# Up projections of two MLPs on one core: seven block products in Strassen's manner in place of eight

## What is computed

```python
qn = q / (norm(q, axis=1) + 1e-06); kn = k / (norm(k, axis=1) + 1e-06)
a = softmax(kn.transpose(0, 2, 1) @ qn / tau)      # 256 x 256 for each batch
x = (v @ a).reshape(12160, 256)
for w_in, w_out in ((moe_w_in, moe_w_out), (moe2_w_in, moe2_w_out)):
    x = np.maximum(x @ w_in, 0.0) ** 2 @ w_out
```

## Time and profile before

| | us |
|---|---|
| median of 3 runs | 2197.58 |
| lowest, highest | 2196.02, 2198.31 |
| the profiled execution | 2196.81 |
| its span, first to last instruction | 2194.7 |
| PE, DVE, ACT busy in the span | 2179.6, 1252.9, 1018.1 |

### The profile page before, as it was taken

One profiled execution on the slowest core, in us unless ns is written; L12 is line 12 of the kernel. 1 busy time (PEld: TensorE's weight loads), 2 busy tenths in 40 slices (PEclk: granted clock), 3 DMA queues, 4 the chain that ended last, 5 costly groups with the idle time before them and its releaser, 6 DMA issues.

```text
span 2194.7 us, 29614 instructions
## 1 busy us (share of the span) xinstructions
PE 2179.6 (99%) x9836; PEld 1826.6 (83%) x9836; DVE 1252.9 (57%) x1875; ACT 1018.1 (46%) x1722; POOL 3.2 (0%) x10
## 2 busy tenths in 40 slices
PE   8999999999999999999999999999999999999998
PEld 7888888888888888888888888888888888888887
DVE  6765555555565555656655555555555555555544
ACT  5554444444444454444544444444444444444443
POOL 0000000000000000000000000000000000000000
PEclk9999999999999999999999999999999999999999
DMA  8310001100011000112111010110110101101001
GB/s 294 96 49 20 19 19 25 33 19 19 19 29 29 19 19 20 33 23 49 37 20 19 1 20 0 19 19 0 19 18 1 19 0 19 19 0 18 10 1 19
DMA packets 215874, 60.94 MB, mean 28 GB/s; under 512 B 199281, under 2 KB 203377, under 8 KB 215825
## 3 DMA queue, kind: packets, MB, share of 16 engines
q1 hardware_dynamic: 215824, 60.31, 11.7%
HBM read 47.84 MB, written 12.45 MB: 27 GB/s over the span
## 4 chain that ended last, share of the span: by engine, by line
PE 99%; DVE 0%; DMA 0%; ACT 0%; issue 0%; DVEq 0%; SPq 0%
PE bank L321 32%; PE bank L323 32%; PE bank L322 32%; PE bank L455 2%; PE bank L402 0%; DMA qk<-in_k 0%; PE bank L416 0%; DVE s_acc L818 0%; PE bank L410 0%; DVE stats L822 0%; DVE rawl L713 0%; DVE out_sb L726 0%; ACT s_acc L592 0%; ACT rawh L521 0%; DVEq L90 0%
## 5 line engine op out<-in xcount | busy, mean ns | idle before, releaser
L747 DVE TENSOR_TENSOR g_sb<-r_sb 128x512 f32<-128x512 f32 (+1 forms) x768 | 527.3, 687 | 896.6 <-ACT r_sb L545 890.4
L545 ACT ACTIVATE r_sb<-bank 128x512 f32<-128x512 f32 (+1 forms) x768 | 456.0, 594 | 1109.3 <-PE bank L323 1102.1
L713 DVE TENSOR_TENSOR gl<-g_sb,gh 128x512 fp32r<-128x512 f32 (+1 forms) x768 | 519.7, 680 | 0.5 <-DVE g_sb L747 0.5
L533 ACT ACTIVATE gh<-r_sb 128x512 fp32r<-128x512 f32 (+1 forms) x768 | 470.7, 619 | 0.0
L321 PE MATMUL bank<-yh,w2h 128*128 128x512 f32 (+1 forms) x768 | 297.8, 388 | 0.0
L321 PE MATMUL bank<-xh,w1h 128*128 128x512 f32 (+1 forms) x768 | 297.4, 387 | 0.0
L322 PE MATMUL bank<-yl,w2h 128*128 128x512 f32 (+1 forms) x768 | 297.4, 387 | 0.0
L322 PE MATMUL bank<-xl,w1h 128*128 128x512 f32 (+1 forms) x768 | 297.4, 387 | 0.0
L321 PE MATMUL bank<-gh,o2h 128*128 128x512 f32 (+1 forms) x768 | 297.3, 387 | 0.0
L323 PE MATMUL bank<-yh,w2l 128*128 128x512 f32 (+1 forms) x768 | 297.3, 387 | 0.0
L323 PE MATMUL bank<-gh,o2l 128*128 128x512 f32 (+1 forms) x768 | 297.3, 387 | 0.0
(11 more groups left out here) (101 smaller groups left out, 1623.8 us busy)
## 6 DMA issues: line engine op xcount, KB each, us to landing
v_sb<-in_v SPq DMA_DIRECT2D x88, 128.0 KB, 3.0
out<-out_sb SPq DMA_DIRECT2D x88, 128.0 KB, 2.5
raw<-in_q SPq DMA_DIRECT2D x22, 256.0 KB, 2.7
raw<-in_k SPq DMA_DIRECT2D x22, 256.0 KB, 3.0
qk<-in_q SPq DMA_DIRECT2D x10, 512.0 KB, 5.2
qk<-in_k SPq DMA_DIRECT2D x10, 512.0 KB, 6.3
w_early<-in_moe_w_in SPq DMA_DIRECT2D x4, 512.0 KB, 6.0
xT<-in_moe_w_out SPq DMA_DIRECT2D x4, 512.0 KB, 3.9
```

Source lines behind the costliest of these rows:

```text
L533: nc.scalar.activation(gh[:, f % SLOTS, 0:n], r_sb[:, f % 2, 0:n], ACT.Square).then_inc(gh_done, 1)
L545: nc.scalar.activation(r_sb[:, f % 2, 0:n], h_ps[f % SLOTS][:, 0:n], ACT.Relu)\
L713: return nc.vector.tensor_tensor(dst, x, as32(hi), ALU.subtract)
L747: nc.vector.tensor_tensor(g_sb[:, f % 2, 0:n], r, r, ALU.mult).then_inc(sq_done, 1)
```

## The change

The kernel is written anew around a product of 2 x 2 blocks. A **unit** is two tiles of tokens (six units to a batch and layer: five of 2 x 512 and one of 2 x 480 tokens), 24 in all. The first layer of both batches comes first, its output goes to HBM (`y_mid`) and comes back for the second layer. SBUF holds the weights of one layer and batch at a time. A unit goes through eight **periods**; a period is one **chunk** of weights: block c of the first 1024 hidden features and block c of the second 1024. Its up product is a 2 x 2 block matrix of weights (128 x 128 blocks) times a 2 x 2 block matrix of activations, done with seven block products in place of eight (the Winograd form of Strassen's): four sums of weight blocks and four of activation blocks are made first, and each product is three matmuls as before. P1, P6, P7 and P4 add up in one bank, `ps_a`, and ACT copies its value out between them, since the partial sums are wanted too; P2 goes to `ps_b`, P5 and P3 to `ps_c`. The blocks are then C11 = P2 + copy 1 and C12 = P3 + copy 2 and C22 = P5 + copy 3 (adds on DVE), and C21 is the bank after P4. Each C is squared with relu, split, and goes down with 6 matmuls into two of four banks `y_ps`.

The four products of `ps_a` stand apart in the period, with down products of the period before and other up products between. Down work of period k-1 runs in period k. Other work is placed in slots of fixed periods (k counts periods, p is its place in the unit, u the unit):

- **weights**: the chunks for the first unit of a layer or batch are prepared one in a period, in periods 0 to 6, 47 to 54 and 95 to 102 (`w_chunk`): fold (4 float32 matmuls, batches only), `combine_w` (4 sums of 128 columns), `split_w` (896 columns, ACT then DVE). The next period's `p1` waits for it. The down weights are split in periods 0 to 7 and 96 to 103, and `d11` waits for them.
- **tokens**: the next unit's v is transposed at p = 2 and 3 and its sums are made at p = 3 and 4, its seven blocks split at p = 4 to 6. A half of v comes in 8 DMAs of 64 KB in place of 4 of 128.
- **batch 1's logits**: at p = 0, 1, 2, 4, 6, 7 of units 1 to 4, as 4 plain float32 matmuls on the unsplit data, added up in PSUM (bank 7) and not in SBUF; the squares are added at p = 2, 4 and 6 as DVE's last item. There is one buffer for q and k, as before.
- no loops: all 192 periods are straight-line code.

The core of the diff (on SyncE, the loads, stores and their places are left out; they are told above):

```diff
-            def up(kind, c, f, n):
-                wait(pe, relu_done, c - SLOTS + 1)
...
-                for cb in range(CB):
-                    cols = slice(f * P, (f + 1) * P)
-                    mm = three(h_ps[f % SLOTS][:, 0:n], wh_[:, cb, cols], wl_[:, cb, cols],
-                               ah[:, cb, 0:n], al[:, cb, 0:n], cb == 0, cb == CB - 1)
-                mm.then_inc(up_done, 1)
+            def product(m, ps, Q, first):
...
+                nc.tensor.matmul(ps[:, 0:n], wsh[:, c, cols], ah, start=first, stop=False, skip_group_check=not first)
+                nc.tensor.matmul(ps[:, 0:n], wsh[:, c, cols], al, start=False, stop=False, skip_group_check=not first)
+                return nc.tensor.matmul(ps[:, 0:n], wsl[:, c, cols], ah, start=False, stop=True,
+                                        skip_group_check=not first)
+            def p1(Q):
+                wait(pe, c21_relu, Q)
...
+                if c == 0:
+                    pe.wait_ge(x_lo, len(PIECES) * (u + 1))
+                if u % PAIRS == 0 and u <= LAYER:
+                    pe.wait_ge(w_lo, (u // PAIRS) * QUADS + c + 1)
+                product(0, ps_a, Q, True).then_inc(p1_done, 1)
+            def p2(Q):
+                wait(pe, c11_added, Q)
+                product(1, ps_b, Q, True).then_inc(p2_done, 1)
+            def p6(Q):
+                pe.wait_ge(p1_copied, Q + 1)
+                product(5, ps_a, Q, False).then_inc(p6_done, 1)
+            def p5(Q):
+                wait(pe, c12_added, Q)
+                product(4, ps_c, Q, True).then_inc(p5_done, 1)
+            def p7(Q):
+                pe.wait_ge(u_copied, Q + 1)
+                product(6, ps_a, Q, False).then_inc(p7_done, 1)
+            def p4(Q):
+                pe.wait_ge(v_copied, Q + 1)
+                product(3, ps_a, Q, False).then_inc(p4_done, 1)
+            def p3(Q):
+                pe.wait_ge(c22_added, Q + 1)
+                product(2, ps_c, Q, False).then_inc(p3_done, 1)
...
+            for k in range(PERIODS + 1):
+                up, dn = k < PERIODS, k > 0
+                if up:
+                    p1(k)
+                if dn:
+                    d11(k - 1)
+                beside(k)
+                if up:
+                    p2(k)
+                    p6(k)
+                if dn:
+                    d22(k - 1)
+                if up:
+                    p5(k)
+                    p7(k)
+                if dn:
+                    d21(k - 1)
+                if up:
+                    p4(k)
+                if dn:
+                    d12(k - 1, 0)
+                    d12(k - 1, 1)
+                if up:
+                    p3(k)
```

ScalarE and VectorE after, each period:

```diff
+                if dn:
+                    square21(k - 1)
+                if up:
+                    copy_p1(k)
+                if dn:
+                    high(k - 1, G21, F21, c21_sq, d21_done, g21_hi)
+                if p == 1 and u > 0:
+                    take_y(u - 1, 1)
+                if dn:
+                    high(k - 1, G12, F12, c12_sq, d12_done, g12_hi)
+                beside_early(k)
+                if up:
+                    copy_u(k)
+                    high(k, G11, F11, c11_sq, d11_done, g11_hi)
+                beside_mid(k)
+                if up:
+                    copy_v(k)
+                if p == 0 and u > 0:
+                    take_y(u - 1, 0)
+                beside_late(k)
+                if up:
+                    relu21(k)
+                    high(k, G22, F22, c22_sq, d22_done, g22_hi)
...
+                if dn:
+                    add12(k - 1)
+                    square(k - 1, F12, c12_added, c12_sq)
+                    g_low(k - 1, G22, F22, g22_hi, g22_lo)
+                if up:
+                    add11(k)
+                    square(k, F11, c11_added, c11_sq)
+                if dn:
+                    g_low(k - 1, G21, F21, g21_hi, g21_lo)
+                    g_low(k - 1, G12, F12, g12_hi, g12_lo)
+                beside_early(k)
+                if up:
+                    g_low(k, G11, F11, g11_hi, g11_lo)
+                beside_mid(k)
+                if up:
+                    add22(k)
+                    square(k, F22, c22_added, c22_sq)
+                beside_late(k)
```

More of the change, by code:

```diff
@@ new lines, in down @@
+            def down(Q, g, half, t, d, first, last):
+                u, c = divmod(Q, QUADS)
+                n = width(u)
+                ps, cols = y_ps[d, t][:, 0:n], slice(d * P, (d + 1) * P)
+                nc.tensor.matmul(ps, oh[:, half, c, cols], gh[:, g, 0:n], start=first, stop=False)
+                nc.tensor.matmul(ps, oh[:, half, c, cols], gl[:, g, 0:n], start=False, stop=False)
+                return nc.tensor.matmul(ps, ol[:, half, c, cols], gh[:, g, 0:n], start=False, stop=last)
@@ new lines, in d22, with d21 @@
+            def d22(Q):
+                u, c = divmod(Q, QUADS)
+                pe.wait_ge(g22_lo, Q + 1)
+                if c == 0:
+                    wait(pe, y1_taken, u)
+                down(Q, G22, 1, 1, 0, c == 0, False)
+                down(Q, G22, 1, 1, 1, c == 0, False).then_inc(d22_done, 1)
+            def d21(Q):
+                c = Q % QUADS
+                pe.wait_ge(g21_lo, Q + 1)
+                down(Q, G21, 1, 0, 0, False, c == QUADS - 1)
+                down(Q, G21, 1, 0, 1, False, c == QUADS - 1).then_inc(d21_done, 1)
@@ new lines, in d12, with raw_logits @@
+            def d12(Q, d):
+                c = Q % QUADS
+                if d == 0:
+                    pe.wait_ge(g12_lo, Q + 1)
+                mm = down(Q, G12, 0, 1, d, False, c == QUADS - 1)
+                if d == 1:
+                    mm.then_inc(d12_done, 1)
+            def raw_logits(m):
+                np_ = TP if m // 2 == FULL else P
+                pe.wait_ge(raw_loaded, 32 * (m + 1))
+                for j in range(2):
+                    for ib in range(CB):
+                        cols = slice(j * C + ib * P, j * C + (ib + 1) * P)
+                        mm = nc.tensor.matmul(ps_t[:, ib * C:(ib + 1) * C], raw[0:np_, 1, cols],
+                                              raw[0:np_, 0, j * C:(j + 1) * C],
+                                              start=m == 0 and j == 0 and ib == 0, stop=m == RAWS - 1 and j == 1,
+                                              skip_group_check=True)
+                mm.then_inc(raw_used, 1)
@@ L399, in norms @@
+            def norms():
                 for n in range(NN):
@@ L535, in stage @@
-            def stage(s, n, before, between):
-                for f in range(NF):
-                    if before is not None and f == before[0]:
-                        take_y(*before[1:])
-                    c = s * NF + f
-                    wait(act, sq_done, c - 1)
-                    wait(act, gh_done, c - 1)
-                    act.wait_ge(up_done, c + 1)
-                    nc.scalar.activation(r_sb[:, f % 2, 0:n], h_ps[f % SLOTS][:, 0:n], ACT.Relu)\
-                        .then_inc(relu_done, 1)
-                    if f:
-                        square(s, f - 1, n)
-                    between(f)
-                square(s, NF - 1, n)
@@ L702, in _ @@
+            take_y(UNITS - 1, 1)
         @block.vector
```

1043 lines of the change are left out of this document (499 added, 544 removed).

## The result

| | before | after |
|---|---|---|
| median of 4 runs, us | 2197.31 | 2143.0 |
| lowest, highest | 2196.02, 2198.31 | 2142.68, 2147.02 |
| the profiled execution, its span | 2196.81, 2194.7 | 2142.68, 2140.8 |

The ratio is 0.9757, 95% interval 0.974 to 0.9774: 2.4% faster, 54 us where 63 were forecast. The forecast was 2134, its range 2098 to 2182.

A forecast was written before the change was run, and what follows sets the result against it. PE's own stream was taken to bound the kernel. Fewer matmuls (-129.5) against added float32 work, waits, loads and end summed to -63.3: span 2131.4, forecast 2134 us, range 2098 to 2182.

The forecast's parts named there:

- MLP matmuls: Up and down products: 45 matmuls a period in place of 48, 2074.2 us falling to 1944.7, -129.5 us.
- periods that prepare weights: In 23 periods the weight split on ACT delays the third copy, P4 0.85 us late; +26.3 us in all, bounds 0 to 45.
- first period: No down work covers the copies and its own chunk must be prepared, at half clock: +5 us (0 to 8).
- loads (raw, v): Batch 1's raw loads 1.75 us late four times, 7 us, plus 1 for the second v tile: +8 us (0 to 20).
- end: After the last matmul: two ACT block copies, eight issues replacing four, a 1.0 us wait for G22: +4 us.
- The ordinary period: Periods without preparation are PE-bound at 10.2 us, third copy 0.45 us ahead of P4; waits cost nothing.
- Rival C: Every ordinary period waits on copies through ACT, 0.25 us over 192 periods: 2182 us (2155 to 2198), chance 0.24.
- Rival E: The straight-line program of 8,700 PE rows is not supplied in time; slower, chance 0.03.
- Rival B: Extra waits are hidden, so weight, first-period and load terms vanish: 2095 us (2090 to 2112), chance 0.15.
- the next p1 waits for DVE's low part, just covered: In weight periods the next P1's wait for DVE's low part of the weights (1.09 us) is just covered.
- clock 1.00 after 75 us: Sign that the forecast is right: PE's granted clock stays at 1.00 once 75 us have passed.
- Rival D: Waits of 1 to 2 us lower the clock; 23 weight periods run half their matmuls at 1.2 GHz: 2252 us, chance 0.08.

The follow-up runs named there:

- experiment 1: Changed kernel with product P2 computed twice in every period, so eight block products in place of seven; 2273.66 us, ratio 1.0348.
- Experiment 2: Changed kernel with the down product d21 moved from before P4 to behind it, leaving the third copy without cover; 2343.55 us, ratio 1.0653.
- experiment 3: Changed kernel with ACT's split of the next weights moved behind the third copy in the 23 weight periods; 2135.17 us, ratio 0.9714.
- experiment 4: Changed kernel with DVE's square sum at p = 6 moved ahead of the late work; 2135.19 us, ratio 0.9719.
- experiment 9: Changed kernel with the last eight of the 16 final stores issued from ACT's queue instead of SyncE's; 2142.09 us, ratio 0.975.
- the six matmuls: Changed kernel with six unused float32 matmuls between the first fold and the first up product, a busy start for PE; 2142.29 us, ratio 0.9749.

## Why the prediction was right, and by how much its steps were off

By spans, forecast and measured, each against the kernel before. The rows of the periods are what PE's starts take over the price list:

| step | forecast | measured |
|---|---|---|
| MLP matmuls | -129.5 | -126.7 |
| logits in float32 | +7.3 | +7.3 |
| folds and start | +14.0 | +14.1 |
| periods that prepare weights | +26.3 | +25.5 |
| first period | +5 | +5.2 |
| loads (raw, v) | +8 | +7.9 |
| second softmax | +1.6 | +1.5 |
| end | +4 | +5.8 |
| clock in period 1 | none | +2.7 |
| fold's weight load behind v | none | +2.7 |
| sum | -63.3 | -54.0 |

The measured span is 2140.8, 53.9 under 2194.7, so that 0.1 have no row.

**The gain.** It is PE's count of matmuls, as experiment 1 shows. The term was off by 2.8: 480 columns take 0.2166, not the 0.215 taken between 448 and 512, over 1440 matmuls 2.3; and twelve in 2.72 us are 0.2267, where I had used 0.2271 (0.5).

**The ordinary period.** Its waits were put at nothing, with 0.45 in hand; the profile has 0.5 in hand and no wait in 860 us. Rival C, which asked for 0.25 a period, is out. Experiment 2 shows how near it stands: one down product, 1.36 us, in another place makes it true in every period. Rival E is out as well, by the same 860 us without a gap; the program has 9196 PE rows, not the 8,700 put there.

**Weight periods.** The place (the third copy behind the split behind DVE's sums), the 23 periods and the size were right: 0.75 a period against 0.85, and 1.43 named at p = 5 where a split of x stands between. Rival B, that ACT's queue hides it, is out: experiment 3 takes the cause away and the waits go. The sets measured 8.3, 7.4 and 9.9 against 8.5, 7.8 and 10.0. The first period took 11.7 us for 6.5 us of work, so 5.2, where the forecast wrote 12 for 6.5 and then +5. The part of the sentence that proved thin is "the next p1 waits for DVE's low part, just covered": it hides no more than it does in this order.

**Loads.** Four waits of 1.79, 1.43, 1.89 and 1.68 against 1.75 each, and experiment 4 confirms the chain; with what is lost around them they cost 7.9. The tile of v cost PE nothing where I had put 1 for it.

**The two terms that weren't there** make over half of the miss of 9.4. For the tile of v I had priced the issues (8 of 64 KB at 0.6; they take 0.505) but had looked only at who waits for v. What is queued behind them in SyncE's queue, batch 1's first weight load, wasn't asked, and it cost 2.7. And the half clock of the start was carried into the first period but not to period 1: the sign "clock 1.00 after 75 us" did not hold, since the stretch 78 to 86 shows 0.58.

**The end.** After the last matmul I counted 8 issues; there are 16 in the one queue, since the two tiles of the last unit are ready together: 11.4 from the last matmul's start where before it took 6.6. Of +4.8 in place of +3, experiment 9 gets 2 back. The last period's wait for the low part of G22, put at 1.0, measured 1.0.

**Rival D** had the clock fall from waits of 1 to 2 us, in up to 23 periods, at 5.1 us each. In kind it was nearer than I put it, in place and size it was wrong. In the changed kernel the waits of the weight periods are named at 0.45 to 1.43, apart from the first of 1.69; one fall stands behind that one and none behind the others. Experiment 2, which makes them 1.68 to 2.79, has falls behind 11 of 23, at some 1.6 us each. So what would have decided against the change was a longer wait than it has, and even then it costs a third of what I took. The Trainium skill, "TensorE: Matmul & The Clock Gate", section "A second HAM failure mode: psum-queue depth-cycling", tells of a kernel whose frequent micro-idles between groups of matmuls made the clock oscillate. Experiment 2 agrees with it in that the clock fell behind 11 of its 23 longer waits; its 169 of 0.66 and 0.69, the frequent ones, left the clock at 1.00, which does not agree.

**What stays open.** What makes the clock fall behind one wait and not behind the next. Behind the wait of 1.68 to 1.70 in the first period it fell in three profiles of seven; behind the wait of 2.53 to 3.00 at the fold in four of six; behind 24 waits for raw loads of 1.26 to 2.18, in six profiles, never; behind the wait of 2.04 that the six matmuls leave ahead of the first up product, in four profiles, never. The forecast can't be sharpened there by more than a chance: some 3 us at either place. Nor is it settled that the busy start takes the second fall away, since it was absent in three profiles that have the wait of 1.68 to 1.70 and no busy start, and in that of experiment 3, where that wait is 0.69. Why the last float32 logits ran at half clock in four profiles is open too.

## What to carry to other kernels
Where a bank is read between two products that add up in it, the margin is the work put between them less the reader's own queue: look at everything that stands before the read on that engine, above all at an item that itself waits for a third engine. The time saved by taking one wait away is bounded by the next wait at the same place, and a gain can be lost again at a later wait for a DMA, here more by the clock behind it than by the wait. For every transfer that is split or moved, ask who is behind it in its queue, not only who waits for it.

## What the runs showed of the hardware that I had not expected
- At full clock the second matmul of 512 columns behind a wait for the third copy starts 0.34 after the first, not 0.227 (rows of the weight period above); behind the waits for `ol` it is 0.31.
- Where float32 matmuls are followed by fp32r ones, the starts shift by -0.20 and then +0.19, with no net loss.
- 480 columns take 0.2166, 512 take 0.2267, 448 take 0.2027: the 32 columns from 448 to 480 cost 0.014, those from 480 to 512 0.010.
- The clock kept its full level through 169 waits of 0.7 us in one kernel and behind the waits of 0.45 to 1.43 in the weight periods of the changed one. Behind waits of 1.68 to 3.00 it fell at some and not at others, for some six to thirteen matmuls at a time; the 7.2 at the start was followed by half clock in every profile that has it.
- Issues of 64 KB in runs of 128 bytes take 0.51 in SyncE's queue and 0.55 in ACT's while both run.
- Of a program of 9196 matmul records without a loop, 1.18 MB through the instruction queue, 860 us ran without a gap.
